# Recurrent attention between dense matmuls: five visits a step, an outer product by head, decays ahead, loads let go in parts

## The reference, cut to what matters

```python
# r, k, v, w: (4 batches, 8 heads, 768 tokens, 48), u: (8, 48)
for t in range(S):
    cur = einsum('bhd,bhe->bhde', u[None] * kt, vt)
    y[:, :, t] = einsum('bhd,bhde->bhe', rt, state + cur)
    state = wt[:, :, :, None] * state + einsum('bhd,bhe->bhde', kt, vt)
x = y as (3072 tokens, 384)
h = x @ w_in;  x = (h * clip(h + 3, 0, 6) / 6) @ w_out        # w_in 384 x 2048, w_out 2048 x 384
h = x @ w_in2; out = (h * sigmoid(h)) @ w_out2
```

## Time and profile before

| | us |
|---|---|
| median of 3 runs | 946.02 |
| lowest and highest | 945.34, 947.06 |
| the profiled execution's own time | 945.16 |
| its span in the trace | 943.4 |
| TensorE busy with matmuls in the span | 916.1 |
| VectorE, ScalarE, GpSimd busy | 457.7, 313.9, 148.8 |

### The profile page before, as it was taken

The page is one execution under the profiler, slowest core; times in us unless marked ns, Lnnn a source line. Parts: engine busy times, 40 slices in busy tenths (PEclk is TensorE's granted clock), DMA queues, the critical chain, the costliest instruction groups (busy, mean ns, idle before and its releaser), DMA issues.

```text
span 943.4 us, 14944 instructions
## 1 busy us (share of the span) xinstructions
PE 916.1 (97%) x5684; PEld 788.7 (84%) x5684; DVE 457.7 (49%) x692; ACT 313.9 (33%) x517; POOL 148.8 (16%) x134
## 2 busy tenths in 40 slices
PE   5679999999999999999999999999999999999998
PEld 4568888888888888888888789999999999999997
DVE  6866646564664656466445643333333333343332
ACT  2343223233223323332244542333332332332332
POOL 6454213321421332142000000000000000000000
PEclk7679999999999999999999999999999999999999
DMA  7561130304113030311203100000000000000000
GB/s 239 189 175 56 56 98 12 109 0 109 54 54 88 20 109 0 109 54 54 100 1 101 67 1 0 15 19 0 33 0 0 33 0 0 33 0 0 34 1 34
DMA packets 13367, 48.54 MB, mean 51 GB/s; under 512 B 1568, under 2 KB 2208, under 8 KB 13344
## 3 DMA queue, kind: packets, MB, share of 16 engines
q1 hardware_dynamic: 13344, 48.23, 16.3%
HBM read 43.50 MB, written 4.72 MB: 51 GB/s over the span
## 4 chain that ended last, share of the span: by engine, by line
PE 93%; DVE 2%; DMA 1%; POOL 1%; issue 1%; ACT 0%; SPq 0%; POOLq 0%; ACTq 0%
PE bank L652 15%; PE bank L653 14%; PE bank L654 14%; PE bank L676 7%; PE bank L678 7%; PE bank L677 7%; PE bank L664 7%; PE bank L666 7%; PE bank L665 7%; PE bank L706 2%; PE bank L732 2%; PE bank L716 2%; PE bank L736 1%; DMA x<-u_row 1%; PE bank L698 1%
## 5 line engine op out<-in xcount | busy, mean ns | idle before, releaser
L652 PE MATMUL bank<-x_hi,w_hi 128*128 (+1 forms) x576 | 230.0, 399 | 1.4 <-DVE x_lo L563 1.4
L654 PE MATMUL bank<-x_hi,w_lo 128*128 (+1 forms) x576 | 227.1, 394 | 0.0
L653 PE MATMUL bank<-x_lo,w_hi 128*128 (+1 forms) x576 | 227.0, 394 | 0.0
L375 ACT CAST g_hi<-g 128x512 fp32r<-128x512 f32 x192 | 119.1, 620 | 286.3 <-PE bank L678 144.3
L491 DVE TENSOR_TENSOR g<-g,bank 128x512 f32<-128x512 f32 x96 | 66.0, 687 | 244.4 <-ACT g L369 244.4
L498 DVE TENSOR_TENSOR g_lo<-g,g_hi 128x512 fp32r<-128x512 f32 x192 | 138.3, 720 | 0.9 <-ACT g_hi L375 0.9
L493 DVE SCALAR_TENSOR_TENSOR g<-g,bank 128x512 f32<-128x512 f32 x96 | 66.0, 688 | 141.3 <-ACT g L367 141.3
L652 PEld LDWEIGHTS bank<-x_hi,w_hi 128*128 128x128 f32 x576 | 108.8, 189 | 27.2 <-issue 4.0
L678 PE MATMUL bank<-w_hi,g_lo 128*128 128x384 f32 x384 | 129.5, 337 | 0.0
L676 PE MATMUL bank<-w_hi,g_hi 128*128 128x384 f32 x384 | 129.5, 337 | 0.0
L677 PE MATMUL bank<-w_lo,g_hi 128*128 128x384 f32 x384 | 128.9, 336 | 0.0
(11 more groups left out here) (89 smaller groups left out, 817.6 us busy)
## 6 DMA issues: line engine op xcount, KB each, us to landing
unit_in<-rkv_tm SPq DMA_DIRECT2D x23, 576.0 KB, 6.5
unit_in<-rk_fm SPq DMA_DIRECT2D x23, 448.0 KB, 4.1
x<-w SPq DMA_DIRECT2D x8, 768.0 KB, 4.9
unit_in<-w SPq DMA_DIRECT2D x8, 768.0 KB, 4.4
unit_in<-w_fm SPq DMA_DIRECT2D x23, 226.2 KB, 2.9
out<-tmp SPq DMA_DIRECT2D x5, 768.0 KB, 3.3
out<-tmp SPq DMA_DIRECT2D x4, 192.0 KB, 2.0
x<-rkv_tm SPq DMA_DIRECT2D x1, 576.0 KB, 12.7
```

The costliest lines, as they stand in the source:

```text
L375: nc.scalar.copy(g_hi[:, p, :], g[:, p, :]).then_inc(ghi_done, 1)
L652: nc.tensor.matmul(h_ps[j % 2][:, :], wh, xh, start=k == 0, stop=False)
L653: nc.tensor.matmul(h_ps[j % 2][:, :], wh, xl, start=False, stop=False)
L654: last = nc.tensor.matmul(h_ps[j % 2][:, :], wl, xh, start=False, stop=k == KT - 1)
```

## The change

- TensorE visits attention in five slots: 4, 7, 10, 12, 14. In visit number b it does the transposes of unit b, the outer product and the values of unit b - 1, then the scores of unit b. The first visit has only transposes and scores, the last only outer product and values. VectorE adds the state of unit b - 1, hands over its `x_lo` and then masks unit b.
- The backward scans are in slots 2, 5, 8, 11, the forward scans with `own` in slots 3, 6, 9, 11.
- The outer product runs by head: eight matmuls of 48 weight columns and 48 moved columns, even heads to partitions 0 to 47, odd ones to 64 to 111 of the same 192 columns.
- The banks: even scores and outer product share `att[0]`, odd scores and transposes `att[1]`, the result has `att[2]`. So the scores of unit b wait for ScalarE's copy of its transposes (`kt_kept`) and for the state additions of unit b - 1 (`added`), and the transposes and the outer product wait for masks.
- A new semaphore `queries_read` is raised behind the 12 query matmuls (in the prologue behind the 12 with the scores). VectorE's state addition waits for it instead of `y_full`.
- Of a unit's loads w waits for the forward scan of the unit that held the place, r/k for its `queries_read`, r/k/v for its `y_full`.
- On GpSimd the decayed queries wait for the forward scan alone; behind them a product of one column (`spin`) takes the waits for `own` and for the values of the unit before, and the diagonal follows.
- In the prologue the pieces keep their order; the outer product, the semaphores and the loads change there too.

```diff
-        run_banks = [[att[0], att[1], att[2], att[2], att[0]]]
+        run_banks = [[att[0], att[1], att[0], att[1], att[2]]]
...
-        RUN_SLOTS = {0: 2, 4: 2, 5: 3, 1: 4, 2: 5, 3: 5}
+        VISITS = [4, 7, 10, 12, 14]
+        SCANS = [2, 5, 8, 11]
+        FORWARDS = [3, 6, 9, 11]
 
         def run_pieces(slot):
-            return [(b, k) for k, first in RUN_SLOTS.items() for b in range(B) if slot == 3 * b + first]
+            pieces = [(b, SCAN) for b in range(B) if SCANS[b] == slot]
+            pieces += [(b, k) for b in range(B) if FORWARDS[b] == slot for k in (FORWARD, OWN)]
+            if slot in VISITS:
+                b = VISITS.index(slot)
+                pieces += [(b, TURN), (b - 1, OUTER), (b - 1, VALUES), (b - 1, STATE), (b, SCORES), (b - 1, XHI), (b - 1, XLO), (b, MASK)]
+            return [(b, k) for b, k in pieces if 0 <= b < B]
...
-                if c is not None or b == 3:
-                    sp.wait_ge(y_full, last + 1)
+                again = c is not None or b == 3
+                if again:
+                    sp.wait_ge(fwd_done, last + 1)
                 sp.dma_start(w, w_fm[bass.ds(step * B + b, 1)].rearrange("o p n -> (o p) n")).then_inc(w_loaded[m], 16)
+                if again:
+                    sp.wait_ge(queries_read, last + 1)
                 sp.dma_start(rk.rearrange("p x i t -> p (x i t)"),
                              rk_fm[bass.ds(step * B + b, 1)].rearrange("o p n -> (o p) n")).then_inc(rk_loaded[m], 16)
+                if again:
+                    sp.wait_ge(y_full, last + 1)
                 sp.dma_start(tm.rearrange("p x d -> p (x d)"),
...
-            def queries_and_diagonal(b, a, c):
+            def old_diagonal_read(b, a, c):
                 pool.wait_ge(own_done, a + 1)
                 pool.wait_ge(y_full, a)
-                decayed_queries(b, a, c)
-                own_diagonal(b, a, c)
+                nc.gpsimd.tensor_tensor(spin[:, :], half[:, :], half[:, :], ALU.mult).then_inc(spun, 1)
...
-                    queries_and_diagonal(b, B * (c + 1) + b, c)
+                    decayed_queries(b, B * (c + 1) + b, c)
+                    old_diagonal_read(b, B * (c + 1) + b, c)
+                    own_diagonal(b, B * (c + 1) + b, c)
...
                         if c is not None:
-                            dve.wait_ge(scaled, 2 * (a - B))
+                            dve.wait_ge(masked, 2 * a)
...
                         else:
-                            dve.wait_ge(y_full, a + 1)
+                            dve.wait_ge(queries_read, a + 1)
                             dve.wait_ge(scaled, 2 * (a - B) + 2)
...
                         if sets == 1:
-                            pe.wait_ge(added, 2 * a)
+                            pe.wait_ge(masked, 2 * a)
...
+                    if k == SCORES:
                         pe.wait_ge(rt_done, a + 1)
                         if sets == 1:
-                            pe.wait_ge(xlo_done, a)
+                            pe.wait_ge(kt_kept, a + 1)
+                            pe.wait_ge(added, 2 * a)
...
-                    if k == 2:
+                    if k == OUTER:
                         pe.wait_ge(kt_kept, a + 1)
-                        if some(2 * (a + 1 - sets)):
+                        if sets == 1:
+                            pe.wait_ge(masked, 2 * a + 2)
+                        elif a + 1 > sets:
                             pe.wait_ge(added, 2 * (a + 1 - sets))
                         pe.wait_ge(tm_loaded[m], 16 * taken(b, c))
-                        for i in range(PAIRS):
-                            last = nc.tensor.matmul(banks[2][0:KROWS, i * 2 * D:(i + 1) * 2 * D], kt_tok[:, i * KROWS:(i + 1) * KROWS],
-                                                    tm[:, 2, i * 2 * D:(i + 1) * 2 * D], start=True, stop=True)
+                        for h in range(H):
+                            q, i = h % 2, h // 2
+                            last = nc.tensor.matmul(banks[2][ODD * q:ODD * q + D, i * D:(i + 1) * D],
+                                                    kt_tok[:, i * KROWS + ODD * q:i * KROWS + ODD * q + D],
+                                                    tm[:, 2, h * D:(h + 1) * D], start=True, stop=True)
                         last.then_inc(outer_full, 1)
```

More of the change, by code:

```diff
@@ L74, in build @@
         half = sb("half", [P, 1])
+        spin = sb("spin", [P, 1])
         def x2_step(c, k):
@@ L150, in build @@
         scaled = sem("scaled")
+        queries_read = sem("queries_read")
         added = sem("added")
@@ L164, in build @@
         diag_done = sem("diag_done")
+        spun = sem("spun")
         v_mid_done = sem("v_mid_done")
@@ L203, in w_chunk @@
             return part[:, (i % CHUNKS) * CHUNK:(i % CHUNKS + 1) * CHUNK]
+        SCAN, FORWARD, OWN, TURN, SCORES, MASK, OUTER, VALUES, STATE, XHI, XLO = range(11)
         def pro_pieces(slot):
-            order = ([(0, 0), (0, 5), (1, 0), (1, 5)] if slot == 0 else
-                     [(slot - 1, 4), (slot - 1, 1), (slot - 2, 2), (slot - 2, 3), (slot + 1, 0), (slot + 1, 5)])
+            order = ([(0, SCAN), (0, FORWARD), (1, SCAN), (1, FORWARD)] if slot == 0 else
+                     [(slot - 1, OWN), (slot - 1, TURN), (slot - 1, SCORES), (slot - 1, MASK),
+                      (slot - 2, OUTER), (slot - 2, VALUES), (slot - 2, STATE), (slot - 2, XHI), (slot - 2, XLO),
+                      (slot + 1, SCAN), (slot + 1, FORWARD)])
             return [(b, k) for b, k in order if 0 <= b < B]
@@ L395, in attention @@
                     rk, w, tm = units[m]
-                    if k == 1:
+                    if k == TURN:
                         act.wait_ge(kt_turned, a + 1)
@@ L406, in attention @@
                         nc.scalar.copy(v_mid_put[b % 2], middle.rearrange("p i (q e) -> p i q e", q=2)).then_inc(v_mid_done, 1)
-                    if k == 3:
+                    if k == XHI:
                         act.wait_ge(y_full, a + 1)
@@ L514, in attention @@
                     p_last = segs(back)[:, :, 0:1]
-                    if k == 0:
+                    if k == SCAN:
                         dve.wait_ge(w_loaded[m], 16 * taken(b, c))
@@ L540, in attention @@
                                                       banks[q][:, :].rearrange("p (h t) -> p h t", h=4)).then_inc(masked, 1)
-                    if k == 4:
+                    if k == OWN:
                         dve.wait_ge(rku_done, a + 1)
@@ L546, in attention @@
                                              tm[:, 0, :].rearrange("p (i q d) -> p i q d", i=PAIRS, q=2), AX.X).then_inc(own_done, 1)
-                    if k == 2:
+                    if k == STATE:
                         if c is None:
@@ L550, in attention @@
                         else:
-                            dve.wait_ge(y_full, a + 1)
+                            dve.wait_ge(queries_read, a + 1)
                             dve.wait_ge(scaled, 2 * (a - B) + 2)
-                        outer = banks[2][:, 0:PAIRS * 2 * D].rearrange("p (i e) -> p i e", i=PAIRS)
+                        outer = banks[2][:, 0:PAIRS * D].rearrange("p (i e) -> p i e", i=PAIRS)
                         for odd in range(2):
@@ L557, in attention @@
                             if c is None:
-                                nc.vector.tensor_copy(st, outer[rows, :, cols]).then_inc(added, 1)
+                                nc.vector.tensor_copy(st, outer[rows, :, :]).then_inc(added, 1)
                             else:
-                                nc.vector.tensor_tensor(st, st, outer[rows, :, cols], ALU.add).then_inc(added, 1)
-                    if k == 3:
+                                nc.vector.tensor_tensor(st, st, outer[rows, :, :], ALU.add).then_inc(added, 1)
+                    if k == XLO:
                         dve.wait_ge(xhi_done, a + 1)
@@ L731, in attention @@
                                 i, e = n // 3, n % 3 * Q
-                                nc.tensor.matmul(region(n), state[b][0:KROWS, i, e:e + Q], rk[:, 0, i, :], start=n < 4, stop=False)
+                                last = nc.tensor.matmul(region(n), state[b][0:KROWS, i, e:e + Q], rk[:, 0, i, :], start=n < 4, stop=False)
+                            last.then_inc(queries_read, 1)
                         for n in range(REGIONS):
@@ L735, in attention @@
                             values = v_mid[b % 2][:, i, 0, :] if e == 1 else tm[:, 2, n * Q:n * Q + Q]
-                            nc.tensor.matmul(region(n), values, scores[:, e // 2 * PAIRS + i, :], start=c is None and n < 4, stop=False)
+                            last = nc.tensor.matmul(region(n), values, scores[:, e // 2 * PAIRS + i, :], start=c is None and n < 4, stop=False)
+                        if c is None:
+                            last.then_inc(queries_read, 1)
                         for n in range(1, REGIONS, 3):
```

6 lines of the change are left out of this document (3 added, 3 removed).

## The result

| | kernel before | kernel after |
|---|---|---|
| median of the runs, us | 945.39 (943.2 to 947.06) | 947.5 (945.81 to 949.68) |
| span of the profiled execution, us | 943.4 | 945.3 |
| ratio of the times, 95% interval | | 1.0023 (1.0012 to 1.0034) |

The change costs 0.23%, some 2.2 us. The forecast was +2.2 us on the median of before (948.2 against 946.02).

The account below looks back on a forecast made before the run. TensorE, busy 97% of the span, was taken as the bound. A step: -1.64 + 0.88 + 0.10 + 1.10 = +0.44 us, five steps +2.2, giving 948.2 us; the 8-in-10 range was 943.0 to 953.5.

Parts of the forecast that it names:

- three inner visits: TensorE's visits in slots 7, 10, 12: 3.93 us each against 4.40, 0.47 less apiece.
- last visit: TensorE's visit with outer product and values alone: 2.44 us against 2.67, 0.23 less a step.
- first wait: First visit of a step: scores wait for ScalarE's copy to kt_tok, 0.88 us a step.
- second wait: Inner visits: scores wait for VectorE's two state additions, 0.05 us in each of two visits, 0.1 a step.
- third wait: Slot 12: unit 3's late decays and turns of GpSimd and VectorE delay scores or transposes, 1.1 us a step (0.4 to 1.3).
- the size of a pair: Outer product: two 48-column passes side by side take 0.05 us (ends 0.03 and 0.10); sixteen passes span 0.40.
- A: Rival: outer product's halves run in turn, a pair costs 0.09 to 0.10 us; +5, 953.2 us; chance 0.15.
- C: Rival: 48-column passes cost less, 0.03 us a pair; 0.4 us a step, 946.2 us; chance 0.10.
- The entry drain of the last visit: Drain of TensorE before the last visit's narrow outer product, not needed by its old form: 0.08 us.
- The order of turns: Slot 11: GpSimd and VectorE exclude each other; whoever waits needs its own length less some 0.14 us once the other ends.
- Rival B: Unit 3 in time: slot 12's wait shrinks to 0.1 to 0.5 us a step; 943.5 us; chance 0.17.
- D: Rival: all gain stays, only the wait for ScalarE's copy remains; 3.8 us less, 942.2 us; chance 0.06.

Follow-up runs that it names:

- e10: Changed kernel with state additions over 8 of 48 columns a head, most of the state left out; 946.08 us, ratio 0.9998 to the kernel before.
- e1: Changed kernel with the first visit's transposes in the result's bank, so scores need not wait for ScalarE's copy; 943.66 us, ratio 0.9973 to the kernel before.
- e4: Changed kernel with the outer product in its old form, four matmuls of 112 weight and 96 moved columns; 953.01 us, ratio 1.0087 to the kernel before.
- e3: Kernel before, its schedule kept, with only the outer product by head in two column halves; 939.75 us, ratio 0.9938 to the kernel before.
- e5: Changed kernel without GpSimd's second product (times u) of each unit, leaving u out of the result; 942.35 us, ratio 0.9972 to the kernel before.
- e6: Changed kernel with token-order r and k loaded in their own earlier transfer, v still waiting for the values; 943.94 us, ratio 0.9977 to the kernel before.
- e2: Changed kernel with the last unit's forward scan in slot 12 and visit in slot 13; 944.03 us, ratio 0.9978 to the kernel before.
- e9: Changed kernel with VectorE's state additions waiting for the end of the values again, not the query passes; 956.92 us, ratio 1.0117 to the kernel before.

## Why the prediction was right, point by point

The total came out at +2.2 us on both sides. The mechanism and its three waits were right, but that the totals agree so closely is luck: the gain was put too low, the second wait at a third of its size, and the two misses cancelled. All times in us a step.

| term | forecast | measured | where |
|---|---|---|---|
| three inner visits | -1.41 | -1.56 | e10, without waits: 3.74 to dense + 0.14 = 3.88 against 4.40 |
| last visit | -0.23 | -0.27 | 2.40 against 2.67 |
| first wait | +0.88 | +0.93 | e1 |
| second wait, slots 7 and 10 | +0.10 | +0.29 | e10 |
| third wait, slot 12, with its share of the second | +1.10 | +1.06 | mean of the five steps |
| sum | +0.44 | +0.45 | +0.44 by the step's length |

The gain was underrated by 0.19, the waits by 0.20. With both right the sum stays the same; with one of them right the forecast would have missed by 1 us in 948.

**The outer product.** The step that failed is the size of a pair, 0.05. The sixteen passes start at 254.94, and the last at 254.94 + 0.56 - 0.21 = 255.29 (a pass of 48 columns is 0.21 in flight), so they span 0.35 (0.357 by the single starts) and not 0.40. The first gap between pairs is 0.08, the six behind it 0.045 each. Rivals A (halves in turn, from 0.055 on) and C (0.03) both fall. C's price of 0.4 us a step doesn't fit the prediction's own 0.25 for each 0.01 a pair either, which makes it 0.5. The Trainium skill, "TensorE: Matmul & The Clock Gate", Part 3, says that a weight load overlaps matmuls in flight only where the row group differs. All sixteen passes have the same rows, 128 of them, and e4 against after has them at half the time of the eight wide ones; and all but the first two of their weight loads, 0.12 us each, run while earlier passes are in flight. Here the measurement decides against that sentence.

**The drains.** The entry drain of the last visit was put at 0.08 and is 0.09. The rest of a seam (0.14 to 0.20) held everywhere.

**The first wait.** The mechanism, its place and its being alone (no copy could be earlier) were right. It is 0.05 more because TensorE starts 0.10 behind the copy's end and not 0.05.

**The second wait.** The chain was right: queries end, additions 0.73, scores. The wake-up was wrong again, 0.15 instead of 0.05, and the array was ready at 2.64, 0.05 earlier than forecast. It is small, but in slots 7 and 10 it came to 0.29 us a step where 0.10 was said, and since it is paid in the third inner visit too, to 0.44 in all. It is most of what keeps the merged visits level with e3.

**The third wait.** Forecast and trace of the second step, both from the first transpose of visit 10 (due at 187.45): first product starts 7.35 and 7.28; g_lo ends 8.9 and 8.85; keys end 12.15 and 11.99; forward scan ends 13.25 and 13.08; additions end 15.85 and 15.54; scores late by 1.05 and 0.80. In steps 3 to 5 the product came 0.02 to 0.46 behind g_lo, and the transposes were late by 0.92 where 1.1 was said; the scores then pay the second wait too. The load as a whole was put right: its landing was 4.3 to 5.1 behind its issue in the five steps, where 4.3 was said. The order of turns, "whoever waits needs its own length less some 0.14", carried the whole term. That rule was read from two collisions in the kernel before. The Trainium skill, "SBUF — State Buffer", section "Who interferes with whom", has it as an exclusive lock held for a whole instruction. This trace agrees: in slot 11 of steps 2 and 3 every instruction of either engine that met another one ended most of its own length behind it. Rival B (unit 3 in time) needed one of them out of the way, and D (only the copy's wait) falls with the second and third wait. e5 and e6 show what it would have been: ratio 0.9972 and 0.9977, where B's 943.5 is 0.9973 of 946.02.

**What cost nothing.** The prologue was put at 0 +- 0.3; the first transposes of the loop are at 72.73 us against 72.97. One execution each can't show more: in e1, e2, e9 and e10, whose prologue is the same as after's, they stand between 71.9 and 73.9. GpSimd's one-column product and VectorE's mask stand in no wait of TensorE's. The visits with no wait were to be 3.8 us; there are none, since each inner visit pays at least the 0.145. That sentence of the prediction was wrong.

**What stays open.** Whether e5 gave back 3.5 us or 4.8 its measurement doesn't settle; its steps (0.66 shorter each) speak for the first. Why a transfer lands in 4.3 us in one step and 4.9 in the next, no run here shows, nor how early a load would have to land for the waits to be gone with both products in slot 11.

## What to carry to other kernels

Take a change that bundles several apart before judging it: here one part in three (the outer product by head, e3) brings 0.6%, and the rest brought waits that took all of it back. When work is moved together, list what shares a bank, a port or a queue with what now stands beside it, and write down the turns with their lengths. A wait of 0.145 us that recurs in each merged visit took back most of the 0.23 that merging saves there; count it with the wake-up that the trace shows, not with none.

## What the runs showed of the hardware that was not expected

- Sixteen fp32 passes of 48 weight and 48 moved columns over 128 rows, two side by side in column halves, need 0.36 us from first to last start. Eight of 112 by 96 need 0.67.
- From the end of an awaited instruction to the start of TensorE's matmul it is 0.10 us behind ScalarE (157.60 to 157.70), 0.13 behind GpSimd (283.73 to 283.86) and 0.15 behind VectorE (257.09 to 257.24).
- Going into the narrow outer product costs 0.09 us, from dense matmuls (e3) as from the transposes (0.48 against 0.39 in e4); going into the wide one costs nothing.
- A landing time that differs by 0.05 us can change which engine has the first turn (product at 7.56, before g_lo, in step 1; at 7.61, behind it, in step 5). The wait then changes its place, from the scores to the transposes. Its size is 0.81 to 1.12 us.
